# Retention and a mixture of experts: 18 chunks of 128 tokens in place of 24 chunks of 96

## The chip, the core and the metric

The kernel runs on one NeuronCore of a Trainium2 chip. The metric is the device time of one execution in microseconds (us), the median over runs. The core has five engines that run side by side and meet only through semaphores: TensorE (PE, matrix products; PEld is its loading of stationary operands), VectorE (DVE), ScalarE (ACT), GpSimd (POOL) and SyncE (SP, which here only issues DMAs). SBUF is the on-chip memory, PSUM the eight banks into which TensorE writes.

## The reference

```
scores = q @ k.T / sqrt(64)                       # 4 batches, 8 heads, 576 tokens, 64 dims
gamma  = 1 - 2 ** (-5 - head)
ret    = scores * (rel >= 0 ? gamma ** rel : 0)   # rel = query position - key position
x      = (ret @ v), heads side by side            # 2304 tokens x 512
logits = x @ w_gate                               # 8 experts
expert = argmax(logits);  gate = 1 / sum(exp(logits - max))
slot of a token = how many tokens before it chose the same expert (capacity 576)
out[token] = gate * relu(x[token] @ w1[expert]) @ w2[expert]     # 512 -> 1024 -> 512
```

The sequences are independent in the retention; the count of the slots runs over all 2304 tokens in order.

## The kernel before

**Retention.** A batch of 576 tokens is cut into NC = 6 chunks of C = 96 tokens. Instead of the whole score matrix the kernel keeps a running state of each head, the sum of k times v over all earlier chunks of the sequence, with k divided by its decay. For chunk c of batch b TensorE does, in this order:

- `inter` (L483, 8 matmuls): state times the decayed q, `qs`; left out where c is 0. It waits for `qs_made` and `state_copied`.
- `intra` (L493, 8): v times the masked scores `probs`. It waits for `masked`.
- `add_state` (L501, 8): scaled k (`k_sc`) times v, added up in PSUM bank 6; left out in the last chunk of a batch.
- `scores` of the next chunk (L469, 8).
- `turn_chunk` (L512, 4 transposes) and `gate_logits` (L519, 4 matmuls of 8 columns against `w_gate`).

Every one of these is a product in full float32, which the profile shows as two matmul records each (transposes: one), so `inter` is x16. The eight matmuls of a group work in pairs on two halves of the array. Moving columns are the tokens of a chunk, except in `add_state` (64) and in the transposes (128); the stationary operand of `scores`, `turn_chunk` and `gate_logits` has as many columns as the chunk has tokens, that of the others 64.

Beside it, GpSimd makes `qs` (L366: q times a decay table `q_dec`, one table for each of the chunk positions, loaded in five DMAs during the first batch) and `k_sc` (L371). VectorE makes `probs` (L860, `mask`: scores in PSUM times a table in `const`, two instructions a chunk) and copies the logits (L864). ScalarE copies x out of PSUM (L732, `xT`), copies the state out of PSUM in two instructions of 64 partitions (L751) and copies the turned x (L738, `x_nat`), which SyncE stores to `x_rows` in DRAM. When a chunk has been turned, SyncE issues the loads of q and k (`qk_raw`) and of k and v (`kv_raw`) of the chunk three ahead, into one of three buffers.

**Routing.** Six chunks make a routing group, here a batch. While the next batch runs, VectorE picks the experts (`pick_expert`), TensorE counts (`count_before`, L528, L531, L534), VectorE makes slots and payloads (`positions`, `pay_rows`, `slots`, `pay_gates`) and TensorE adds the group to a map of slots (`make_map`, L545). The last group is routed in two parts, four chunks early and two after the end of the retention, and ends in index tables.

**Experts.** Then GpSimd gathers the rows of each expert, and each expert runs 16 blocks of 12 matmuls (L634 to L636), its weights split by ScalarE (L727) and VectorE (L851) into a high and a low part. This stage follows from the routing alone.

**Loops.** `by_batch` writes out the first and the last batch and runs batches 1 and 2 in one loop with registers. The order on each engine is the order of the code.

Of the kernel before, what the change touches and what calls it, by code (L numbers as in the profile page):

```python
# [35 lines left out]
ZERO_STEPS = 12  # L36
# [18 lines left out]
K_RANK = K_DK + NC * HEADS  # L55
# [7 lines left out]
def shape_constants():  # L63

    gamma = 1.0 - 2.0 ** (-5.0 - np.arange(HEADS))
    pos = np.arange(SEQ).reshape(NC, C).T
# [7 lines left out]
    k[:, K_IOTA:K_ALL] = np.arange(CAP)  # L74
    k[:, K_DK:K_RANK] = (gamma ** -pos[:, :, None].astype(np.float64)).reshape(C, -1)
# [7 lines left out]
    qd = gamma[head][:, None, :, None] ** np.arange(SEQ) / np.sqrt(DH)  # L83
    qd = np.broadcast_to(qd, (2, DH, PAIRS, SEQ)).reshape(128, PAIRS, NC, C).transpose(0, 2, 1, 3)
# [9 lines left out]
def by_batch(eng, body):  # L94

    body(0, True, False)
    with eng.Fori(1, BATCH - 1) as b:
        body(b, False, False)
    return body(BATCH - 1, False, True)
# [20 lines left out]
def retention_moe(nc, qk, kv, w_gate, w1, w2, consts, qdecay, eye, out):  # L120
# [6 lines left out]
    with ExitStack() as ctx:  # L127
# [25 lines left out]
        with ExitStack() as one:  # L153
# [7 lines left out]
            q_dec = s1("q_dec", [128, NC, PAIRS, C])  # L161
# [60 lines left out]
        q_dec_in = [sem(f"q_dec_in{c}") for c in range(NC)]  # L222
# [64 lines left out]
        def _(sp):  # L287
            def load_chunk(b, c):
                sp.dma_start(qk_raw[:, c % 3], qk[b, c]).then_inc(qk_in[c % 3], 16)
                sp.dma_start(kv_raw[:, c % 3], kv[b, c]).then_inc(kv_in[c % 3], 16)  # L290
# [13 lines left out]
            def load_decay(c):  # L304
                sp.dma_start(q_dec[:, c], qdecay[:, c]).then_inc(q_dec_in[c], 16)

            sp.dma_start(qk_raw[:, 0], qk[0, 0]).then_inc(qk_in[0], 16)
            sp.dma_start(const[:, 0:K_RANK], consts[:, 0:K_RANK]).then_inc(const_in, 16)
            sp.dma_start(kv_raw[:, 0], kv[0, 0]).then_inc(kv_in[0], 16)
            sp.dma_start(qk_raw[:, 1], qk[0, 1]).then_inc(qk_in[1], 16)  # L310
# [7 lines left out]
            def batch(b, first, last):  # L318
                for c in range(NC):

                    sp.wait_ge(x_turned, b * NC + c + 1)
                    if not (last and c + 3 >= NC):
                        load_chunk(b + (c + 3) // NC, (c + 3) % NC)
                    sp.wait_ge(x_copied, b * NC + c + 1)
                    sp.dma_start(x_rows[bass.ds((b * NC + c) * C, C), :], x_nat[:, c % 2, :]
                                 ).then_inc(x_stored[c % 2], 16)
                    if first and c + 3 < NC:
                        load_decay(c + 3)
# [6 lines left out]
            by_batch(sp, batch)  # L335
# [14 lines left out]
        def _(pool):  # L350
# [7 lines left out]
            def scale_chunk(b, c):  # L358
                n = b * NC + c

                wait(pool, x_made, n - 1)
                wait(pool, state_made, b * (NC - 1) + max(c - 1, 0))
                if c > 0:
                    pool.wait_ge(q_dec_in[c], 16)
                    pool.wait_ge(qk_in[c % 3], 16 * (2 * b + c // 3 + 1))
                    pool.tensor_tensor(qs[:, c % 2], qk_raw[:, c % 3, 0], q_dec[:, c], ALU.mult  # L366
                                       ).then_inc(qs_made, 1)
                if c < NC - 1:
                    pool.wait_ge(kv_in[c % 3], 16 * (2 * b + c // 3 + 1))
                    decay = const[:, K_DK + c * HEADS:K_DK + (c + 1) * HEADS].unsqueeze(2).broadcast_to((C, HEADS, DH))  # L370
                    pool.tensor_tensor(k_sc[:, c % 2], kv_raw[:, c % 3, 0], decay, ALU.mult).then_inc(k_scaled, 1)  # L371
# [757 lines left out]
```

## Time and profile before

| | us |
|---|---|
| median of 3 runs | 385.71 |
| lowest, highest | 381.7, 389.11 |
| the profiled execution | 387.06 |
| its span, first to last instruction | 385.1 |
| TensorE busy | 358.6 |
| VectorE busy | 214.5 |
| ScalarE busy | 186.8 |
| GpSimd busy | 135.0 |

A row of the timeline or of the chain of waits begins with start and length in us from the span's start. In the chain, the pieces lie end to end: each is what the end of the kernel waited for at that moment. A row of a stretch gives its length, the busy time of each engine with the number of its instructions, the granted TensorE clock, the DMA engines' busy share and GB/s.

### The profile page before, as it was taken

What the parts mean: (1) busy time and instruction counts of PE and PEld (TensorE: products, weight loads), DVE (VectorE), ACT (ScalarE), POOL (GpSimd) and SP (SyncE); (2) the same over time, 40 slices, a digit from 0 to 9 for tenths busy, and PEclk for the clock granted to TensorE, in tenths of its full rate; (3) what the DMA queues carried; (4) which work ended last, traced back from release to release, by engine and by line L of the source; (5) the groups of instructions that cost most, each with busy time, mean ns of one, the idle gap of its engine ahead of it and who ended that gap; (6) DMA issues with size and microseconds to landing.
All of it is one profiled execution on the core that took longest, in us unless ns stands there. A gap on an engine that the chain in (4) does not pass through costs nothing.

```text
span 385.1 us, 10982 instructions
## 1 busy us (share of the span) xinstructions
PE 358.6 (93%) x3594; PEld 338.4 (88%) x3595; DVE 214.5 (56%) x450; ACT 186.8 (48%) x367; POOL 135.0 (35%) x131
## 2 busy tenths in 40 slices
PE   8999999999999799499899999989999999998993
PEld 4998888999976599399899999989999999998992
DVE  3145545838774475356456556646756757754741
ACT  1344343436431365266365447547657646655641
POOL 3675344534506223025205504522542541321323
PEclk9999999999995999799999999999999999999999
DMA  8789987887963599815635544654663664550101
GB/s 240 222 267 270 307 248 216 248 255 218 272 192 109 185 386 372 311 61 190 196 111 176 167 163 129 202 184 136 204 220 136 202 211 136 197 163 4 60 0 56
DMA packets 27435, 73.41 MB, mean 191 GB/s; under 512 B 7114, under 2 KB 7882, under 8 KB 27408
## 3 DMA queue, kind: packets, MB, share of 16 engines
q1 hardware_dynamic: 21008, 63.57, 51.2%
q0 software_dynamic: 6400, 9.46, 8.2%
q8 instruction: 18, 0.29, 0.3%
q14 instruction: 9, 0.07, 0.1%
HBM read 64.61 MB, written 19.92 MB: 220 GB/s over the span
## 4 chain that ended last, share of the span: by engine, by line
PE 85%; issue 5%; DVE 3%; DMA 3%; POOL 2%; ACT 1%; POOLq 0%; another core or an unknown queue 0%; DVEq 0%; ACTq 0%; SPq 0%
PE bank L634 18%; PE bank L636 18%; PE bank L635 17%; PE bank L469 5%; PE bank L483 4%; PE bank L493 4%; PE bank L519 4%; PE bank L512 3%; PE bank L627 3%; PE bank L622 3%; PE bank L501 2%; DMA qk_raw<-in_qk 2%; PE bank L572 1%; DMA x_gat<-x_rows,slot_row 1%; PE bank L545 1%
## 5 line engine op out<-in xcount | busy, mean ns | idle before, releaser
L634 PE MATMUL bank<-m_hi,w_hi 128*128 x512 | 155.1, 303 | 6.5 <-DVE w_lo L851 3.2
L635 PE MATMUL bank<-m_hi,w_lo 128*128 x512 | 153.7, 300 | 0.0
L636 PE MATMUL bank<-m_lo,w_hi 128*128 x512 | 153.1, 299 | 0.0
L851 DVE TENSOR_TENSOR w_lo<-w_raw,w_hi 128x512 fp32r<-128x512 f32 x128 | 89.0, 695 | 37.2 <-ACT w_hi L727 33.6
L634 PEld LDWEIGHTS bank<-m_hi,w_hi 128*128 128x128 f32 x512 | 96.2, 188 | 10.1 <-issue 10.1
L635 PEld LDWEIGHTS bank<-m_hi,w_lo 128*128 128x128 f32 x512 | 96.2, 188 | 0.0
L636 PEld LDWEIGHTS bank<-m_lo,w_hi 128*128 128x128 f32 x512 | 96.2, 188 | 0.0
L727 ACT ACTIVATE w_hi<-w_raw 128x512 fp32r<-128x512 f32 x128 | 79.6, 625 | 25.0 <-PE bank L636 21.1
L388 POOL DMA_INDIRECT out<-y_nat,slot_row x40 | 41.7, 1042 | 133.6 <-PE bank L636 87.1
L1030 DVE SCALAR_TENSOR_TENSOR m_lo<-bank,m_hi 128x384 fp32r<-128x384 f32 x64 | 35.7, 558 | 38.8 <-ACT m_hi L809 35.8
L382 POOL DMA_INDIRECT x_gat<-x_rows,slot_row x37 | 40.4, 1093 | 46.2 <-PE bank L636 27.5
L809 ACT ACTIVATE m_hi<-bank 128x384 fp32r<-128x384 f32 x64 | 31.5, 492 | 40.8 <-PE bank L636 37.5
L860 DVE TENSOR_TENSOR probs<-bank,const 96x384 f32<-96x384 f32 x48 | 24.4, 548 | 40.5 <-PE bank L469 40.4
L366 POOL TENSOR_TENSOR qs<-qk_raw,q_dec 128x384 f32<-128x384 f32 x20 | 20.8, 1039 | 34.8 <-DMA qk_raw<-in_qk 21.8
L732 ACT ACTIVATE xT<-bank 128x384 f32<-128x384 f32 x24 | 11.8, 490 | 39.1 <-PE bank L493 39.1
L788 ACT ACTIVATE y_sb<-bank 128x384 f32<-128x384 f32 x32 | 15.7, 491 | 30.4 <-PE bank L636 27.2
L371 POOL TENSOR_TENSOR k_sc<-kv_raw,const 96x512 f32<-96x512 f32 x20 | 20.8, 1041 | 19.9 <-DMA kv_raw<-in_kv 19.9
L738 ACT ACTIVATE x_nat<-bank 96x512 f32<-96x512 f32 x24 | 14.2, 592 | 25.6 <-PE bank L512 23.0
L1042 DVE TENSOR_TENSOR y_sb<-bank,y_sb 128x384 f32<-128x384 f32 x32 | 17.8, 557 | 13.3 <-PE bank L636 11.1
L766 ACT ACTIVATE m_hi<-bank 128x512 f32 (+1 forms) x24 | 13.3, 598 | 24.2 <-PE bank L622 13.9
L1026 DVE TENSOR_TENSOR m_lo<-bank,m_hi 128x512 f32 (+1 forms) x24 | 15.5, 687 | 16.7 <-ACT m_hi L766 15.5
L469 PE MATMUL bank<-qk_raw 64*96 64x96 f32 x384 | 23.7, 266 | 0.7 <-DMA qk_raw<-in_qk 0.7
(89 smaller groups left out, 360.7 us busy)
## 6 DMA issues: line engine op xcount, KB each, us to landing
w_raw<-in_moe_w SPq DMA_DIRECT2D x64, 512.0 KB, 3.3
qk_raw<-in_qk SPq DMA_DIRECT2D x24, 384.0 KB, 4.7
kv_raw<-in_kv SPq DMA_DIRECT2D x24, 384.0 KB, 5.3
x_rows<-x_nat SPq DMA_DIRECT2D x24, 192.0 KB, 4.5
out<-zeros SPq DMA_DIRECT2D x12, 384.0 KB
q_dec<-in_qdecay SPq DMA_DIRECT2D x5, 192.0 KB, 5.2
out<-y_nat,slot_row POOLq DMA_INDIRECT x40, 2.7
x_gat<-x_rows,slot_row POOLq DMA_INDIRECT x37, 2.9
```

The lines of the kernel that those rows point to most:

```text
L366: pool.tensor_tensor(qs[:, c % 2], qk_raw[:, c % 3, 0], q_dec[:, c], ALU.mult).then_inc(qs_made, 1)
L382: pool.indirect_dma_start(out=dst[:, g, :], out_offset=None, in_=x_rows[:, :], in_offset=bass.IndirectOffsetOnAxis(ap=slot_row[:, g, e:e + ...
L388: pool.indirect_dma_start(out=out[:, :], out_offset=bass.IndirectOffsetOnAxis(ap=slot_row[:, g, e:e + 1], axis=0), in_=y_nat[:, g, :], in_ ...
L469: last = pe.matmul(score_ps[0:C, u, p * C:(p + 1) * C], qk_raw[r, c % 3, 1, p, :], qk_raw[r, c % 3, 0, p, :], start=True, stop=True, skip_ ...
L634: pe.matmul(dst, w_hi[:, s, i, :], hi[:, i, cols], start=(i == 0), stop=False)
L635: pe.matmul(dst, w_lo[:, s, i, :], hi[:, i, cols], start=False, stop=False)
L636: last = pe.matmul(dst, w_hi[:, s, i, :], lo[:, i, cols], start=False, stop=(i == K4 - 1))
L727: act.activation(w_hi[:, j % SLOTS], w_raw[j // 2][:, j % 2 * 512:j % 2 * 512 + 512].rearrange("p (k n) -> p k n", k=K4), ACT.Copy).then_i ...
L809: last = act.activation(m_hi[:, H0 + j, 0:WA], ring[j % SLOTS][:, 0:WA], ACT.Relu)
L851: dve.tensor_tensor(w_lo[:, j % SLOTS], w_raw[j // 2][:, j % 2 * 512:j % 2 * 512 + 512].rearrange("p (k n) -> p k n", k=K4), w_hi[:, j % S ...
L860: dve.tensor_tensor(probs[:, u], src, decay[:, u], ALU.mult).then_inc(masked, 1)
L1030: return dve.scalar_tensor_tensor(out=m_lo[:, H0 + f, cols], in0=src, scalar=0.0, in1=m_hi[:, H0 + f, cols].bitcast(f32), op0=ALU.max, op1 ...
```

## The change

The chunk grows from 96 to 128 tokens, so that 2304 tokens are 18 chunks. 576 is 4.5 x 128, so the chunks run over sequence ends: nine chunks (`PERIOD`) hold two sequences, and in the fifth of them (`MID`, chunks 4 and 13) the first 64 tokens end one sequence and the last 64 begin the next. There the mask is made in three pieces per half (a memset of zeros, 64 rows x 4x64, and 64 rows x 512), `inter` takes 64 columns only, and the state starts anew. `inter` is left out in chunks 0 and 9, `add_state` in chunks 8 and 17.

Six chunks are still a routing group, so there are three groups instead of four. The group loop is written out in full on every engine.

`q_dec` becomes one table of 128x512 for all chunks, loaded once; what a chunk's start adds to the decay is put into the state: VectorE multiplies the state by a column of `const` while it copies it from PSUM (`scale_state`, two instructions of 64x4x64), and ScalarE's state copies go. The first load of `const`, for which the mask and `k_sc` wait, becomes 128x1132 elements.

```diff
-C = 96
-NC = SEQ // C
+C = 128
+CHUNKS_ALL = TOKENS // C
+NC = 6
+GROUPS = CHUNKS_ALL // NC
+PERIOD = 2 * SEQ // C
+MID, HALF = SEQ // C, SEQ % C
...
-ZERO_STEPS = 12
+ZERO_STEPS = 9
...
-            q_dec = s1("q_dec", [128, NC, PAIRS, C])
+            q_dec = s1("q_dec", [128, PAIRS, C])
...
-            load_decay(1)
-            sp.dma_start(kv_raw[:, 1], kv[0, 1]).then_inc(kv_in[1], 16)
-            load_chunk(0, 2)
-            load_decay(2)
...
+            sp.dma_start(q_dec[:, :, :], qdecay).then_inc(q_dec_in, 16)
+            sp.dma_start(kv_raw[:, 1], kv[1]).then_inc(kv_in[1], 16)
+            load_chunk(2)
...
-                    if first and c + 3 < NC:
-                        load_decay(c + 3)
...
-            def scale_chunk(b, c):
-                n = b * NC + c
-
+            def scale_chunk(n):
+                c = n % PERIOD
                 wait(pool, x_made, n - 1)
-                wait(pool, state_made, b * (NC - 1) + max(c - 1, 0))
+                wait(pool, state_made, with_state(n - 2))
                 if c > 0:
-                    pool.wait_ge(q_dec_in[c], 16)
-                    pool.wait_ge(qk_in[c % 3], 16 * (2 * b + c // 3 + 1))
-                    pool.tensor_tensor(qs[:, c % 2], qk_raw[:, c % 3, 0], q_dec[:, c], ALU.mult
+                    cols = slice(0, HALF if c == MID else C)
+                    if n == 1:
+                        pool.wait_ge(q_dec_in, 16)
+                    pool.wait_ge(qk_in[n % 3], 16 * (n // 3 + 1))
+                    pool.tensor_tensor(qs[:, n % 2, :, cols], qk_raw[:, n % 3, 0, :, cols], q_dec[:, :, cols], ALU.mult
                                        ).then_inc(qs_made, 1)
...
-                    if c < NC - 1:
-
-                        act.wait_ge(state_made, b * (NC - 1) + c + 1)
-                        if first and c == 0:
-                            act.wait_ge(zero_made, 2)
-                        for u in range(2):
-                            r = slice(64 * u, 64 * u + 64)
-                            last_copy = act.activation(state[r, :, r], state_ps[r, :, :], ACT.Copy)
-                        last_copy.then_inc(state_copied, 1)
-                    copy_x(b, c)
+                    copy_x(n)
...
+                parts = ((slice(0, C), slice(0, C)),)
+                if n % PERIOD == MID:
+                    parts = ((slice(0, HALF), slice(0, HALF)), (slice(HALF, C), slice(0, C)))
                 for u in range(2):
-                    src = score_ps[0:C, u, 0:PAIRS * C].rearrange("c (a i) -> c a i", a=PAIRS)
-                    dve.tensor_tensor(probs[:, u], src, decay[:, u], ALU.mult).then_inc(masked, 1)
+                    if n % PERIOD == MID:
+                        dve.memset(probs[0:HALF, u, :, HALF:C], 0.0)
+                    for rows, cols in parts:
+                        src = score_ps[rows, u, :].rearrange("c (a i) -> c a i", a=PAIRS)[:, :, cols]
+                        last = dve.tensor_tensor(probs[rows, u, :, cols], src, decay[rows, u, :, cols], ALU.mult)
+                    last.then_inc(masked, 1)
+
+            def scale_state(n):
+
+                start = K_SS + (n + 1) % PERIOD * PAIRS
+                dve.wait_ge(state_made, with_state(n))
+                for u in range(2):
+                    r = slice(64 * u, 64 * u + 64)
+                    last = dve.tensor_tensor(state[r, :, r], state_ps[r, :, :],
+                                             const[r, start:start + PAIRS].unsqueeze(2).broadcast_to((64, PAIRS, DH)),
+                                             ALU.mult)
+                last.then_inc(state_copied, 1)
...
+                    if n % PERIOD < PERIOD - 1:
+                        scale_state(n)
+                return link
```

TensorE's queue in the first batch, before the change: `inter`, `intra`, `add_state`, then the next chunk's `scores`, the transposes and the logits (the shape is output partitions x moving columns).

```order
L483 MATMUL bank<-qs,state 64x96 x8
L493 MATMUL bank<-probs,kv_raw 64x96 x8
L501 MATMUL bank<-kv_raw,k_sc 64x64 x8
L469 MATMUL bank<-qk_raw 96x96 x8
L512 MATMUL bank<-ident,xT 96x128 x4
L519 MATMUL bank<-wg,xT 96x8 x4
```

The same queue in the changed kernel, from the end of chunk 3 through chunk 4, the one over a sequence end.

```order
L529 MATMUL bank<-wg,xT 128x8 x4
L492 MATMUL bank<-qs,state 64x64 x8
L502 MATMUL bank<-probs,kv_raw 64x128 x8
L511 MATMUL bank<-kv_raw,k_sc 64x64 x8
L476 MATMUL bank<-qk_raw 128x128 x8
L522 MATMUL bank<-ident,xT 128x128 x4
L529 MATMUL bank<-wg,xT 128x8 x4
L492 MATMUL bank<-qs,state 64x128 x8
```

The order of a chunk's work stands as it was; what is wider is the moving side of three groups and the stationary side of three.

VectorE's queue before, in the second and third chunk of the first batch: masks and the copy of the logits of the chunk before.

```order
L860 TENSOR_TENSOR probs<-bank,const 96x384 x2
L864 COPY logits<-bank 96x8
L860 TENSOR_TENSOR probs<-bank,const 96x384 x2
L864 COPY logits<-bank 96x8
L860 TENSOR_TENSOR probs<-bank,const 96x384 x2
```

VectorE's queue in the changed kernel, from chunk 2 to the end of chunk 4's mask.

```order
L868 TENSOR_TENSOR probs<-bank,const 128x512 x2
L884 COPY logits<-bank 128x8
L877 TENSOR_TENSOR state<-bank,const 64x4x64 x2
L868 TENSOR_TENSOR probs<-bank,const 128x512 x2
L884 COPY logits<-bank 128x8
L877 TENSOR_TENSOR state<-bank,const 64x4x64 x2
L865 MEMSET probs 64x4x64
L868 TENSOR_TENSOR probs<-bank,const 64x4x64
L868 TENSOR_TENSOR probs<-bank,const 64x512
L865 MEMSET probs 64x4x64
L868 TENSOR_TENSOR probs<-bank,const 64x4x64
L868 TENSOR_TENSOR probs<-bank,const 64x512
```

Two state instructions have come in between the logits' copy of one chunk and the mask of the next; where a chunk has routing work (from the second group on), that work stands ahead of them.

## Rows read from the trace of the kernel before

**Rows 1.** The page's first part: busy time, share of the span, instructions.

```profile
PE 358.6 (93%) x3594; PEld 338.4 (88%) x3595; DVE 214.5 (56%) x450; ACT 186.8 (48%) x367; POOL 135.0 (35%) x131
```

**Rows 2.** Stretches: length, PE, PEld, DVE, ACT, POOL busy; clock, DMA share, GB/s.

```profile
0.00:18.50 18.50, 16.75 (x134) 12.32 (x137) 4.10 (x9) 4.13 (x9) 9.24 (x14) 1.00 0.78 224
18.50:110.50 92.00, 88.83 (x1640) 83.08 (x1636) 55.27 (x165) 39.91 (x89) 40.48 (x37) 1.00 0.86 254
110.50:131.00 20.50, 17.24 (x120) 11.49 (x120) 9.75 (x39) 4.42 (x8) 7.68 (x8) 0.75 0.46 137
131.00:385.00 254.00, 235.74 (x1704) 231.55 (x1704) 145.34 (x238) 138.31 (x262) 77.63 (x73) 0.98 0.50 170
```

**Rows 3.** Chain of waits, one chunk of the last batch: start, length, piece.

```profile
91.19 0.81 PE bank L483 x16
92.00 0.66 PE bank L493 x16
92.66 0.47 PE bank L501 x16
93.12 0.85 PE bank L469 x16
93.97 0.57 PE bank L512 x4
94.55 0.60 PE bank L519 x8
```

**Rows 4.** Chain of waits: a cold chunk's piece, a stall, map, batch start, count.

```profile
16.03 1.28 PE bank L493 x16
...
32.27 0.47 issue
...
84.25 0.97 PE bank L545 x9
...
87.27 0.88 PE bank L493 x16
...
89.47 0.15 PE bank L528
...
90.10 0.48 PE bank L512 x4
```

**Rows 5.** Waits, 0 to 131 us: engine, line, waited for, total, times, longest.

```profile
PE bank L469 <- DMA qk_raw<-in_qk: 0.7, 1, 0.7
...
PE bank L528 <- DVE onehot L896: 0.9, 2, 0.6
```

**Rows 6.** Groups by line and shape: out<-in, count, busy us, mean ns, idle before.

```profile
L860 DVE TENSOR_TENSOR probs<-bank,const 96x384 f32<-96x384 f32 x48 | 24.4, 548 | 40.5 <-PE bank L469 40.4
...
L1026 DVE TENSOR_TENSOR m_lo<-bank,m_hi 128x512 f32 x21 | 13.4, 686 | 14.6 <-ACT m_hi L766 14.5
...
L751 ACT ACTIVATE state<-bank 64x256 f32<-64x256 f32 x40 | 15.1, 378 | 1.7 <-PE bank L501 1.5
...
L371 POOL TENSOR_TENSOR k_sc<-kv_raw,const 96x512 f32<-96x512 f32 x20 | 20.8, 1041 | 19.9 <-DMA kv_raw<-in_kv 19.9
L366 POOL TENSOR_TENSOR qs<-qk_raw,q_dec 128x384 f32<-128x384 f32 x20 | 20.8, 1039 | 34.8 <-DMA qk_raw<-in_qk 21.8 <-DMA q_dec<-in_qdecay 8.9 <-PE bank L501 4.1
```

**Rows 7.** Timeline, VectorE and GpSimd side by side: start, length, instruction.

```profile
37.36 1.04 POOL L371 TENSOR_TENSOR k_sc<-kv_raw,const 96x512 f32<-96x512 f32 x1 [0.43 <-DMA kv_raw<-in_kv]
37.50 0.96 DVE L896 TENSOR_TENSOR onehot<-ranked,r_max 96x48 bf16<-96x48 f32 x1
```

**Rows 8.** Two stretches with full DMA queues, and the page's row on a load.

```profile
36.30:49.00 12.70, 11.76 (x225) 11.07 (x224) 8.27 (x30) 5.00 (x13) 5.11 (x6) 1.00 1.02 311
...
141.00:151.00 10.00, 9.76 (x78) 9.55 (x77) 7.25 (x12) 5.76 (x12) 5.34 (x5) 1.00 1.00 357
...
qk_raw<-in_qk SPq DMA_DIRECT2D x24, 384.0 KB, 4.7
```

**Rows 9.** Timeline at the start: first k_sc and first intra.

```profile
7.17 1.03 POOL L371 TENSOR_TENSOR k_sc<-kv_raw,const 96x512 f32<-96x512 f32 x1 [4.62 <-DMA kv_raw<-in_kv]
...
8.46 1.55 PE L493 MATMUL bank<-probs,kv_raw 96*64 96x96 f32 x16
```

More of the change, by code:

```diff
@@ L91, in wait, with by_group, with_state @@
         eng.wait_ge(sem, value)
[L94 to L99, printed above, removed]
+def by_group(body):
+    for g in range(GROUPS):
+        link = body(g, g == 0, g == GROUPS - 1)
+    return link
+def with_state(n):
+    return n + 1 - (n + 1) // PERIOD
 def by_count(eng, count, body, large, sizes=None):
@@ L221, in retention_moe @@
         out_zeroed = sem("out_zeroed")
-        q_dec_in = [sem(f"q_dec_in{c}") for c in range(NC)]
+        q_dec_in = sem("q_dec_in")
         gate_in = sem("gate_in")
@@ L334, in batch @@
                         load_weights(0, c)
-            by_batch(sp, batch)
+            by_group(group)
             sp.wait_ge(xs_tr, 2 * NA)
@@ L580, in _, with group @@
             pe.wait_ge(scores_cleared, 1)
-            scores(0, 0)
+            scores(0)
             keep_warm(1)
-            def batch(b, first, last):
+            def group(b, first, last):
                 for c in range(NC):
                     n = b * NC + c
-                    inter(b, c)
-                    intra(b, c)
-                    if c < NC - 1:
-                        add_state(b, c)
-                    elif not first and not last:
+                    inter(n)
+                    intra(n)
+                    if n % PERIOD < PERIOD - 1:
+                        add_state(n)
+                    if c == NC - 1 and not first and not last:
                         make_map(b - 1)
-                    if not (last and c == NC - 1):
-                        scores(b + (c + 1) // NC, (c + 1) % NC)
+                    if n + 1 < CHUNKS_ALL:
+                        scores(n + 1)
                     if not first and c == 0:
@@ L732, in copy_xT, with copy_x, group @@
                 act.activation(xT[:, :, :], xT_ps, ACT.Copy).then_inc(xT_copied, 1)
-            def copy_x(b, c):
-                act.wait_ge(x_turned, b * NC + c + 1)
-                wait(act, x_stored[c % 2], 16 * (b * NC // 2 + c // 2))
-                act.activation(x_nat[:, c % 2, :], x_ps[0:C, :], ACT.Copy).then_inc(x_copied, 1)
-            def batch(b, first, last):
+            def copy_x(n):
+                act.wait_ge(x_turned, n + 1)
+                wait(act, x_stored[n % 2], 16 * (n // 2))
+                act.activation(x_nat[:, n % 2, :], x_ps[0:C, :], ACT.Copy).then_inc(x_copied, 1)
+            def group(b, first, last):
                 for c in range(NC):
@@ L759, in batch @@
                         w_high(0, 2 * c + 1)
-            by_batch(act, batch)
-            act.wait_ge(dif_made, BATCH + 1)
+            by_group(group)
+            act.wait_ge(dif_made, GROUPS + 1)
             act.activation(l_exp[:, :, :], l_dif[:, :, :], ACT.Exp).then_inc(exp_made, 1)
@@ L965, in cast_tables, with group @@
                 dve.wait_ge(const_cast, 4)
-            def batch(b, first, last):
+            def group(b, first, last):
+                link = None
                 for c in range(NC):
```

144 lines of the change are left out of this document (75 added, 69 removed).

## The prediction

> **What bounds the kernel now.** I read the busy shares first: TensorE is busy for 358.6 of 385.1 us, VectorE for 214.5 [rows 1]. Then the stretches. The retention runs to about 110.5 us, the last routing to 131, the experts to the end; in the 92 us from 18.5 to 110.5 TensorE is busy for 88.8 us and the DMA engines for 86% at 254 GB/s [rows 2]. So in the stage that the change touches TensorE sets the pace and the DMA engines come second. The experts (254 us) keep their code and data, and I take them as unchanged. Last the chain of waits. One warm chunk is six pieces of TensorE without a gap: 0.81 + 0.66 + 0.47 + 0.85 + 0.57 + 0.60 = 3.96 us [rows 3]. Up to about 18.5 us the same pieces take almost twice that, `intra` 1.28 us for 0.66 [rows 4, 3]: TensorE is at its lower clock there, whatever the clock column says for a stretch without a record. The stalls in the chain are small: 0.47 us without a visible waiter at 32.27, where `inter` stands ready and its last input, `qs`, had itself waited for a table `q_dec` [rows 4, 6]; 0.9 us for the one-hot of VectorE; 0.7 us once for a `qk_raw` load [rows 5].
>
> **The change, part by part.**
>
> *Wider chunks on TensorE.* `intra` and `add_state` have equal tiles and differ in moving columns, 96 against 64: 0.66 against 0.47 us [rows 3]. So 32 columns on eight matmuls cost 0.19 by the difference and 0.22 in proportion; I take 0.21. From it, at 128:
> `inter` 0.81 + 0.21 = 1.02; `intra` 0.66 + 0.21 = 0.87; `add_state` stays 0.47 (it moves 64 columns still; only the contraction is longer); the transposes stay 0.57, plus 0.01 for a wider first load. `scores` moves and loads 128 for 96: 0.85 + 0.21 = 1.06 if only moving columns count, 1.13 if all of it scales by 4/3; I take 1.11. `gate_logits` moves 8 columns only, so its 0.60 is weight loads of 96 columns: 0.60 if a load's time does not grow, 0.80 at 4/3; no row shows wide loads of this kind alone, and I take 0.80, since with 8 moving columns nothing else is left to fill the time.
> A chunk is then 1.02 + 0.87 + 0.47 + 1.11 + 0.58 + 0.80 = 4.85 us, 22% longer for 33% more tokens. The gain is what does not grow: `add_state`, the transposes, and the first latency of each group.
> Before: 24 x 3.96 = 95.0, less four `inter` and four `add_state` (0.81 + 0.47), plus 0.22 at each batch's start, where `intra` takes 0.88 for 0.66 [rows 4]: 90.8. After: 18 x 4.85 = 87.3; chunks 0 and 9 save 1.02 - 0.22 each, chunks 8 and 17 save 0.47 each, chunks 4 and 13 have an `inter` of 64 columns, 0.60, and save 0.42 each: 87.3 - 1.6 - 0.9 - 0.8 = 84.0. **Gain 6.8 us.** With loads that cost nothing it would be 6.8 + 18 x 0.25 = 11.3; with all four scaled groups and the transposes at 4/3 a chunk is 4.94 + 0.18, and the gain 2.0.
>
> *One routing group less.* A map costs 0.97 us, a count 90.10 - 89.47 = 0.63 less the 0.09 that the next transpose is shorter [rows 4]. **Gain 1.5.**
>
> *Stalls that go.* One `q_dec` in place of five tables that come with the chunks: the 0.47 at 32.27 goes. The one-hot was late because VectorE works on it for some 2.1 us after a chunk's logits while TensorE needs only `intra`, `add_state`, `scores` to reach the count; after, an `inter` comes first (the group starts at chunks 6 and 12 are not sequence starts) and the pieces are longer, 3.5 us in all: the 0.9 goes [rows 5]. The load stall of 0.7 may stay. **Gain 1.4.**
>
> *The state on VectorE.* ScalarE's two copies of 378 ns leave a queue that is not on the path. VectorE gets two of 256 elements: its time from PSUM is 548 ns at 384 and 686 at 512 [rows 6], so some 420 at 256, 0.8 a pair; the masks go from 548 to 686 each, about 1.3 a pair. From the end of `add_state` to the next `inter` TensorE has 1.11 + 0.58 + 0.80 = 2.5 us of other work, VectorE needs 0.9: hidden by 1.6 us. The next mask may start when `scores` are done, 1.1 us after `add_state`, just when the state is finished; `intra` comes 0.58 + 0.80 + 1.02 = 2.4 us later and the mask needs 1.3. Behind routing work: the one-hot chain (2.1) plus state (0.8) ends 2.9 us after the logits, where `inter` comes at 4.85. In the last group a chunk has up to 2.1 of gates and a weight split of 0.7 (rows of VectorE's kind at 686 ns [rows 6]) ahead of its state: 3.7, still ahead of 4.85. What takes this cover away is GpSimd: the one-hot of 0.2 us took 0.96 where it met `k_sc` (37.36 to 38.40), ending when that ended [rows 7]. A split that meets `qs` (1.04 x 4/3 = 1.4 us) gives up to 1.4 once or twice in the last group. I put 0 to 3 us in all, and take 0.6.
>
> *The middle chunks.* Two memsets and four products replace two: 2 x (0.2 + 0.4 + 0.6) = 2.4 us, and chunk 4's `intra` comes 0.58 + 0.80 + 0.60 = 2.0 us after its scores. A stall of 0.4 to 0.5, at chunk 4; chunk 13 has a count (0.6) between and hides it. **Loss 0.5.**
>
> *Loads.* A chunk brings 0.52 + 0.52 + 0.26 = 1.31 MB per 4.85 us, 270 GB/s, for 0.98 MB per 3.96 us before, 248. The queues have carried 311 and 357 GB/s when full [rows 8]. A load has the time of two chunks less the pieces after `scores`, about 8.0 us for 6.6 before, and took 4.7 [rows 8]; 4/3 of it is 6.3. No change, with 0 to 8 us as the bounds (below).
>
> *Start and tail.* The first `k_sc` waits for `kv_raw` at 7.17, the first `intra` runs at 8.46 behind warming matmuls [rows 9]. Before it must land 1.60 MB for 1.08; at the 360 GB/s of a full queue that is 1.5 us later, 8.6, so 0.2 is lost. In the part at the lower clock both kernels work without a break, about six warm microseconds each. The tail's `xT` copy and logits grow by 0.3. **Loss 0.5.**
>
> Sum: 6.8 + 1.5 + 1.4 - 0.6 - 0.5 - 0.5 = 8.1 us. The profiled execution took 387.06, so it would take 379.0; it lies 1.35 above the median of 385.71, so the median becomes 377.6, which I round to 377.5.
>
> A rule that speaks against the move of the state is in the Trainium skill, "TensorEngine Tiling (Array Packing)", Performance Considerations, PSUM Bottleneck: use both ScalarE and VectorE to empty PSUM. By that rule VectorE is the next bound, which is the third rival below.
>
> **The rivals.**
> - *The DMA engines bind.* Against my figure of 270 GB/s stands their 86% at 254 GB/s [rows 2], which extrapolates to 295 at full. If they could in truth give no more than now, the stage's 23.4 MB take 92 us as before, and all that is left is nothing to 2 us of routing: 384 to 386. At 295 they take 79 us and do not bind on average, but loads come late in bursts (the two weight loads of the first group): 2 to 4 us, 380 to 382. For it: 0.7 us of it are there already [rows 5]. Against: 311 and 357 [rows 8]. Chance 0.25, most of it the mild form.
> - *Loads of weights don't grow* with the columns, or the wider groups start sooner: up to 4.5 us more gain, 373. Chance 0.12.
> - *VectorE binds (slower).* Each chunk's `inter` or `intra` waits for VectorE because state, split and masks are held by GpSimd. It cancels the gain from 8.1 / 18 = 0.45 us of stall per chunk; slower by 2% needs 0.9 us in every chunk, 393.4. The cover of 1.6 us and of 1.1 us speaks against it. Chance 0.07.
> - *The clock.* The part at the lower clock ends at about 18.5 us now; every microsecond that it lasts longer costs half of that. If TensorE falls back to it in the retention for 10 us, 5 us are lost: 382.5. Nothing between 18.5 and 110.5 shows it [rows 2]. Chance 0.06.
>
> **How the numbers follow.** My forecast has the remaining 0.50. Its own range is 375 to 380.5. With the rivals, 372.5 to 384 leaves out about 2 in 10. Faster by over 2%, about what a measurement of this kernel can tell from no change, is below 378.0: the better half of the forecast and the second rival, 0.54 with the runs' scatter. Within 2%: 0.39. Slower: 0.07.
>
> **What would show it.** In the profile after: chunk pieces of about 1.02, 0.87, 0.47, 1.11, 0.58, 0.80 in the chain, the retention done near 102 us; no wait for `q_dec` or for the one-hot; a mask wait at chunk 4 only; DMA share near 0.9. Wrong if a chunk takes 5.3 us or more (all scales by 4/3), if waits for `qk_raw` or for `state_copied` come in many chunks, or if the experts' 254 us move by more than 2.

## The result, and the profile after

The change takes the median from 385.71 to 372.46 us: ratio 0.969, 95% interval 0.962 to 0.977. The forecast was 377.5, in the range 372.5 to 384. So the direction was right and the gain, 13.2 us, is well over the 8.1 that the sum gave. The ratio is of the fast runs alone (one of the old kernel's five was slow), and by it the gain is 11.8 us and the new time 373.9. That is inside the range, while the plain median, 372.46, lies on its lower edge. The profiled execution took 374.73 (span 372.9) beside 387.06 (span 385.1) before, and the difference of these two spans, 12.2 us, is what the rows below can account for.

The page of the kernel after, busy time (as [rows 1]) and its row on the load of q and k (as the last of [rows 8]):

```profile
PE 348.2 (93%) x3178; PEld 330.3 (89%) x3179; DVE 219.1 (59%) x447; ACT 168.2 (45%) x314; POOL 129.1 (35%) x123
...
qk_raw<-in_qk SPq DMA_DIRECT2D x18, 512.0 KB, 4.7
```

Stretches of the kernel after (columns as in [rows 2]: PE, PEld, DVE, ACT, POOL, clock, DMA share, GB/s):

```profile
0.00:18.50 18.50, 16.48 (x176) 12.80 (x179) 7.79 (x16) 3.90 (x7) 11.05 (x16) 1.00 0.88 317
18.50:96.00 77.50, 74.66 (x1180) 70.11 (x1178) 54.94 (x154) 20.25 (x36) 33.38 (x28) 1.00 0.83 273
96.00:118.00 22.00, 18.93 (x127) 13.18 (x123) 10.06 (x41) 4.91 (x9) 7.20 (x7) 0.69 0.45 136
118.00:372.90 254.90, 238.09 (x1704) 234.15 (x1704) 146.27 (x238) 139.13 (x262) 77.43 (x73) 0.97 0.50 169
```

The retention ends near 96 us and not near 102; the two stages behind it are slightly longer than before (22.0 for 20.5, 254.9 for 254.0). A warm chunk in the chain of waits of the kernel after, to be read against [rows 3]:

```profile
53.90 1.09 PE bank L476 x16
54.99 0.59 PE bank L522 x4
55.58 0.79 PE bank L529 x8
56.38 1.02 PE bank L492 x16
57.40 0.87 PE bank L502 x16
58.27 0.47 PE bank L511 x16
```

These are `scores`, transposes, `gate_logits`, `inter`, `intra`, `add_state`: 4.83 us for the forecast 4.85, each piece within 0.02. TensorE's waits in the retention (8.3 to 96 us), line, what it waited for, total, times, longest:

```profile
PE bank L502 <- DVE probs L868: 2.6, 4, 1.2
...
PE bank L492 <- DVE state L877: 0.4, 1, 0.4
```

There is no wait for `q_dec`, for the one-hot or for a load any more; in their place `intra` waits for VectorE's masks four times (0.28 of the 2.6 us is the very first one) and `inter` once for the state.

**Where the 12.2 us lie.** I cut both spans at three places that both kernels pass: the start of the `intra` of the chunk that begins at token 384 (chunk 4 before, chunk 3 after; 384 is a multiple of both sizes), the last matmul of the last `intra`, and the experts' first product with `w_hi`. The forecast column sorts the prediction's own terms into the same parts.

The two rows on which the first part rests, before and after:

```profile
28.94 0.83 PE L493 MATMUL bank<-probs,kv_raw 96*64 96x96 f32 x16
...
23.25 1.04 PE L502 MATMUL bank<-probs,kv_raw 128*64 128x128 f32 x16
```

| part | before | after | gained | forecast |
|---|---|---|---|---|
| to the `intra` at token 384 | 28.94 | 23.25 | 5.7 | 1.1 |
| from it to the last `intra` | 80.78 | 72.76 | 8.0 | 8.0 |
| to the experts' first matmul | 21.42 | 21.96 | -0.5 | -1.1 |
| experts | 253.9 | 254.9 | -1.0 | 0 |
| span | 385.1 | 372.9 | 12.2 | 8.0 |

(Forecast: 4 chunks of 3.96 against 3 of 4.85 are 1.3, less 0.2 at the start; 19 chunk steps against 14 are 6.2, a group 1.5, stalls +1.4 and -1.1; the last chunk's wider pieces 0.8 and the tail 0.3.) The steady part is right as a sum. The gain that was not forecast is in the first quarter of the retention. The expert row flatters the change: a second trace of the old kernel has 251.1 us there, without the 3.2 us of waits for `w_lo` that the first one has, and against it the new kernel's experts are 3.8 us longer.

### The profile page after: what moved, and what is told of

The parts are those of the page before. It is cut to its first block, busy times and chain, and to the rows that moved or that the text cites. A ratio compares the mean times of both kernels' runs of the same rounds, so it can differ in the third digit from the quotient of the medians.

```text
span 372.9 us, 9780 instructions
## 1 busy us (share of the span) xinstructions
PE 348.2 (93%) x3178; PEld 330.3 (89%) x3179; DVE 219.1 (59%) x447; ACT 168.2 (45%) x314; POOL 129.1 (35%) x123
## 4 chain that ended last, share of the span: by engine, by line
PE 89%; DVE 4%; issue 4%; DMA 1%; ACT 1%; POOL 1%; POOLq 0%; DVEq 0%; ACTq 0%
PE bank L644 20%; PE bank L645 19%; PE bank L646 19%; PE bank L476 5%; PE bank L502 4%; PE bank L632 4%; PE bank L492 4%; PE bank L529 3%; PE bank L637 3%; PE bank L522 2%; DVE probs L868 2%; PE bank L511 2%; PE bank L582 2%; DMA y_nat<-x_rows,slot_row 1%; DVE y_sb L1065 1%
## 5 line engine op out<-in xcount | busy, mean ns | idle before, releaser
L395 POOL DMA_INDIRECT out<-y_nat,slot_row x40 | 40.1, 1002 | 137.9 <-PE bank L646 106.1
L389 POOL DMA_INDIRECT x_gat<-x_rows,slot_row x37 | 41.3, 1118 | 43.6 <-PE bank L646 18.1
L868 DVE TENSOR_TENSOR probs<-bank,const 128x512 f32<-128x512 f32 (+2 forms) x40 | 25.1, 660 | 8.8 <-PE bank L476 8.6
L742 ACT ACTIVATE xT<-bank 128x512 f32<-128x512 f32 x18 | 10.7, 597 | 42.9 <-PE bank L502 42.9
L373 POOL TENSOR_TENSOR qs<-qk_raw,q_dec 128x512 f32<-128x512 f32 (+1 forms) x16 | 19.8, 1236 | 27.9 <-DMA qk_raw<-in_qk 20.4
L877 DVE TENSOR_TENSOR state<-bank,const 64x256 f32<-64x256 f32 x32 | 13.5, 422 | 18.3 <-PE bank L511 18.0
L748 ACT ACTIVATE x_nat<-bank 128x512 f32<-128x512 f32 x18 | 10.7, 597 | 29.3 <-PE bank L522 29.3
L476 PE MATMUL bank<-qk_raw 64*128 64x128 f32 x288 | 21.8, 293 | 0.0
```

The costliest lines, as they stand in the source:

```text
L389: pool.indirect_dma_start(out=dst[:, g, :], out_offset=None, in_=x_rows[:, :], in_offset=bass.IndirectOffsetOnAxis(ap=slot_row[:, g, e:e + ...
L395: pool.indirect_dma_start(out=out[:, :], out_offset=bass.IndirectOffsetOnAxis(ap=slot_row[:, g, e:e + 1], axis=0), in_=y_nat[:, g, :], in_ ...
L476: last = pe.matmul(score_ps[0:C, u, p * C:(p + 1) * C], qk_raw[r, n % 3, 1, p, :], qk_raw[r, n % 3, 0, p, :], start=True, stop=True, skip_ ...
L868: last = dve.tensor_tensor(probs[rows, u, :, cols], src, decay[rows, u, :, cols], ALU.mult)
```

## The experiments

### At the start: the clock, the loads or the tables

Before, TensorE was at its lower level (1.2 GHz) until 18.5 us: its matmuls take twice as long [rows 4]. After, the record of the granted clock steps to the full level at 7.6 us, and the first `intra` is at full speed from the start. Timeline of the kernel after, its first `intra` (before it took 1.55 [rows 9]):

```profile
8.70 1.09 PE L502 MATMUL bank<-probs,kv_raw 128*64 128x128 f32 x16 [0.28 <-DVE probs L868]
```

The new kernel's warming matmuls run on 128 rows and not 96, so that was the first suspect. One run gives the old kernel wide warming, one the new kernel narrow warming.

```diff
-        zeros = sb("zeros", [C, TOKENS // ZERO_STEPS // C * D])
+        zeros = sb("zeros", [128, TOKENS // ZERO_STEPS // C * D])
...
-                    pe.matmul(unused[0:C, 0:n], zeros[:, 0:C], zeros[:, 0:n], start=True, stop=True,
+                    pe.matmul(unused[0:128, 0:n], zeros[:, 0:128], zeros[:, 0:n], start=True, stop=True,
```

> The kernel before, with nothing changed but its warming products of zeros: they use 128 rows and 128 columns of the array in place of 96 and 96 (the tile of zeros is 128 partitions high). Theory A1 (the wider warming products raise the clock earlier): the clock is up near 8 us instead of 18.5, first intra at 8.5, and 4 to 5 us are saved, ratio 0.987. Theory A2 (the wider chunk's own products do it) or B (luck): the rise stays at about 18.5 us or moves in either direction over executions, ratio 1.00.

Measured: 387.1 us, ratio 1.002 (0.998 to 1.007). The clock rose at 5.4 us (at 6.4 in a second trace), and the kernel gained nothing.

```diff
-                    pe.matmul(unused[0:C, 0:n], zeros[:, 0:C], zeros[:, 0:n], start=True, stop=True,
+                    pe.matmul(unused[0:96, 0:n], zeros[0:96, 0:96], zeros[0:96, 0:n], start=True, stop=True,
```

> The changed kernel with its warming products cut back to 96 rows and 96 columns. Theory A1: the clock rises later than 12 us and 3 to 5 us are lost against after_again. Theory A2: the rise stays near 8 us and nothing is lost, within 1 us of after_again.

Measured: 376.74 us, ratio 0.973 (0.964 to 0.981), beside 375.89 for the unchanged new kernel on the same chip. The clock rose at 8.9 us: narrow warming does not hold it down. So wide warming goes with an early rise in the old kernel, but the new one doesn't need it, and by itself it is worth nothing in time.

> The changed kernel unchanged, for its scatter. Theory A (the clock's early rise comes with the change): the clock is up before 12 us again, the warm chunk is 4.82 us again, chunks 4 and 13 stall on VectorE again, ratio to the kernel before 0.962 to 0.977. Theory B (the early rise was luck of that execution): the clock rises anywhere from 7 to 19 us, and the time is up to 5 us longer when it is late.

Measured: 375.89 us, ratio 0.975 (0.969 to 0.980); the clock rose at 6.5 us, the `intra` at token 384 came at 23.00.

A further run makes only one half of the change: chunks stay at 96, but there is one decay table, and VectorE puts the chunk's start into the state.

```diff
-                sp.dma_start(q_dec[:, c], qdecay[:, c]).then_inc(q_dec_in[c], 16)
+            sp.dma_start(q_all[:, :], qdecay).then_inc(q_dec_in, 16)
...
-                                last_copy = act.activation(state[r, :, r], state_ps[r, :, :], ACT.Copy)
+                    last = dve.tensor_tensor(state[r, :, r], state_ps[r, :, :],
+                                             starts[r, at:at + PAIRS].unsqueeze(2).broadcast_to((64, PAIRS, DH)),
+                                             ALU.mult)
```

> The kernel before with only the second half of the change: one decay table for q, and VectorE multiplies the state by the decay of a chunk's start while it copies it. Chunks stay 96 tokens, loops and groups stay. Theory: TensorE's pieces stay 3.96 us a chunk, the 0.47 us at 32 us goes, VectorE's state copy is hidden outside the routing chunks and costs 0 to 2 us in the last batch: ratio 0.997 to 1.005, clock rise at about 18.5. Rival (VectorE binds): 0.4 us or more in most of the 20 chunks with a state, ratio over 1.02.

Measured: 389.41 us, ratio 1.007 (1.002 to 1.011). The clock rose at 8.6 us with narrow warming and narrow chunks.

What each of these gave at the start can be read from 9 to 20 us (columns as in [rows 2]). The kernel before:

```profile
9.00:20.00 11.00, 11.00 (x132) 10.44 (x128) 1.94 (x5) 3.28 (x8) 6.20 (x5) 1.00 0.78 224
```

Before with wide warming, and from its timeline an `inter` and the `qs` that it waited for:

```profile
9.00:20.00 11.00, 9.46 (x170) 8.65 (x170) 2.36 (x6) 3.90 (x9) 5.54 (x5) 0.96 1.04 257
...
16.51 0.99 POOL L366 TENSOR_TENSOR qs<-qk_raw,q_dec 128x384 f32<-128x384 f32 x1 [2.96 <-DMA q_dec<-in_qdecay]
17.60 0.88 PE L483 MATMUL bank<-qs,state 128*64 128x96 f32 x16 [1.28 <-issue]
```

96-token chunks with one table:

```profile
9.00:20.00 11.00, 10.38 (x197) 9.63 (x194) 5.06 (x13) 2.65 (x5) 7.65 (x7) 1.00 1.04 257
```

The kernel after:

```profile
9.00:20.00 11.00, 11.00 (x185) 10.51 (x183) 4.62 (x11) 2.88 (x5) 9.50 (x8) 1.00 0.96 336
```

In the first row TensorE is busy all the time but at the lower clock (132 matmul records in 11 us), and in this trace the DMA engines have slack, 0.78 (a second trace of the old kernel has 0.97 there, and TensorE idles in neither). Once the clock is up the old kernel's demand outruns them: 257 GB/s at a share of 1.04, and TensorE idles 1.5 us of 11, 1.28 of it at once, behind `qs` behind a table. A second trace of that kernel has 4.2 us in three such waits before token 384. So the lower clock hid slow loads, and the earlier clock alone gave nothing in the total. Without four of the five tables (0.8 MB) the idle time falls to 0.6 us. The wide kernel moves 336 GB/s in the same stretch and never waits. The `intra` at token 384 comes at 28.94 in the old kernel (29.96 in another trace of it), 27.76 (with a fall of the clock on the way, 19.0 to 22.4 us) and 29.53 with wide warming, 25.49 with one table, 23.25 with the whole change.

So of the 5.7 us some 3.5 go with the earlier clock and the fewer table bytes together (the clock alone gave nothing in the total; fewer bytes at the lower clock had no run), and some 2.2 with the wide chunks, 1.3 of that TensorE's own. These shares are rough: each stands on one or two traces, and the two of the old kernel differ by 1.0 us.

### The experts

TensorE waits twice for "issue" inside the experts, at the first transposes of an expert, where the old kernel waits once. Waits from 118 us on, kernel after:

```profile
PE bank L632 <- issue: 8.3, 2, 5.6
```

The same in the kernel before (from 131 us; its L622 is the same operation):

```profile
PE bank L622 <- issue: 5.6, 1, 5.6
```

The diff doesn't touch that stage, but it writes the group loop out in full on every engine. One run does that alone to the kernel before:

```diff
-    body(0, True, False)
-    with eng.Fori(1, BATCH - 1) as b:
-        body(b, False, False)
-    return body(BATCH - 1, False, True)
+    for b in range(BATCH):
+        link = body(b, b == 0, b == BATCH - 1)
+    return link
```

> The kernel before with only its loop over batches 1 and 2 written out, as the change does it. Theory: registers and branches cost TensorE the stalls without a waiter near 51 and 60 us, 0.9 us, so 0.5 to 1.5 us faster than before, ratio 0.997. Rival (nothing of the gain comes from the loops): ratio 1.000 within its interval; or more instructions to fetch cost up to 1 us.

Measured: 389.25 us, ratio 1.017 (1.008 to 1.026), 5.9 us over the old kernel's 383.39 on the same chip, where 0.5 to 1.5 us less was expected. Its waits from 117 us on, on the corresponding line:

```profile
PE bank L621 <- issue: 8.1, 2, 5.6
```

The second stall is there, in a kernel that differs only in the written-out loop; the kernels with the loop written out have it (7.3 to 8.4 us in two waits; one further below, which routes its tokens otherwise, has the second wait on another line), the five traces of looped 96-token kernels have one, of 5.5 to 5.9. What the extra stall is, the timeline of the kernel after shows, and its DMA queues from 180 to 186 us:

```profile
185.17 2.18 PE L632 MATMUL bank<-ident,x_gat 128*128 128x128 f32 x9 [2.70 <-issue]
...
q8 instruction: 2, 0.03, 2.0%
```

The expert's transposes start 2.7 us late, and two packets of instructions arrive in that stretch, the second of them from 184.2 us on, just ahead of the stall's end. A second trace of the old kernel has one such packet at its corresponding place, 193 to 199 us:

```profile
q8 instruction: 1, 0.02, 1.2%
```

The Trainium skill, "Runtime: NRT & Kernel Launch", Instruction fetch mechanics, says that instructions come in blocks of 16 KiB and that a taken branch to a target outside the window stalls until the block has come, and prefers full unrolling for that. The trace agrees with the block size (0.03 MB in two packets) and with a stall where the expert loop starts again; the advice did not hold here, since unrolling one loop brought a stall in another. That TensorE waited for that packet, and that the code's place against the blocks decides it, is argued; the runs show only that the stall comes with the written-out loop. Behind it the granted clock falls to half for 3.4 us in the kernel after (185.1 to 188.5 us, mean 0.50), another 1.7 us at most. In the old kernel with the loop written out the retention was 1.5 us longer too, with 2.3 us of waits for `qk_raw` for 0.7 [rows 5]; why, no run shows. Beside the second trace of the old kernel (span 382.1 for 387.6) its retention is 1.3 us longer and its experts 4.3, which is nearly the whole 5.9; the stall is 2.5 of the 4.3, and further short waits for "issue" are 1.6.

### VectorE: the state and the middle chunks

The stall at chunk 4 in the chain of waits of the kernel after, from `scores` to `intra`:

```profile
24.76 1.12 PE bank L476 x16
25.97 0.27 DVE probs L865
26.26 0.42 DVE probs L868
26.69 0.69 DVE probs L868
27.49 0.27 DVE probs L865
27.77 0.42 DVE probs L868
28.20 0.71 DVE probs L868
28.91 0.14 issue
29.05 1.09 PE bank L502 x16
```

The mask in three pieces per half runs 2.94 us from end to end. TensorE's other work is `turn_chunk`, `gate_logits` and a 64-column `inter`, and `intra` is 1.2 us late. Chunk 13 repeats it, and chunk 14 follows. Timeline, kernel after:

```profile
73.66 1.09 PE L502 MATMUL bank<-probs,kv_raw 128*64 128x128 f32 x16 [0.91 <-DVE probs L868]
...
75.36 1.27 POOL L373 TENSOR_TENSOR qs<-qk_raw,q_dec 128x512 f32<-128x512 f32 x1 [2.72 <-PE bank L511]
75.47 1.70 DVE L852 TENSOR_TENSOR w_lo<-w_raw,w_hi 128x512 fp32r<-128x512 f32 x1
77.10 0.85 DVE L877 TENSOR_TENSOR state<-bank,const 64x256 f32<-64x256 f32 x2
78.09 1.09 PE L492 MATMUL bank<-qs,state 128*64 128x128 f32 x16 [0.40 <-DVE state L877]
...
79.41 1.09 PE L502 MATMUL bank<-probs,kv_raw 128*64 128x128 f32 x16 [0.22 <-DVE probs L868]
```

The late mask pushes logits, positions and the weight split `w_lo` behind it; `w_lo` meets GpSimd's `qs` and takes 1.70 us for 0.70; the state after it is late by 0.4 and the next mask by 0.2. In one run the middle chunks are masked like any other (the zeros between the two sequences are left out):

```diff
-                if n % PERIOD == MID:
-                    parts = ((slice(0, HALF), slice(0, HALF)), (slice(HALF, C), slice(0, C)))
...
-                    if n % PERIOD == MID:
-                        dve.memset(probs[0:HALF, u, :, HALF:C], 0.0)
```

> The changed kernel with chunks 4 and 13 masked like all others, two products a chunk (the zeros between two sequences are left out of the mask). Theory: the two stalls of 1.2 and 0.9 us that the traces show before intra of chunks 4 and 13 go, and chunk 14's with them: 2 to 3 us faster than after_again, ratio 0.968. Rival (the stalls are made up for behind, as TensorE is fed by others later): under 1 us.

Measured: 370.18 us, ratio 0.967 (0.961 to 0.973). From the first `intra` to the last matmul of the last it takes 84.65 us, for 87.31 and 87.05 in the two traces of the unchanged kernel without a clock fall in that stage; and one mask wait of 0.4 us is left. So the middle chunks cost 2.4 to 2.7 us, their followers counted, where the forecast had 0.5.

The other half of the question is the state. Here ScalarE copies it, as before, without the decay of the chunk's start:

```diff
+                        for u in range(2):
+                            r = slice(64 * u, 64 * u + 64)
+                            last_copy = act.activation(state[r, :, r], state_ps[r, :, :], ACT.Copy)
...
-                    if n % PERIOD < PERIOD - 1:
-                        scale_state(n)
```

> The changed kernel with the state copied by ScalarE in two instructions as before, and not multiplied by the decay of a chunk's start (this part of the computation is left out). It frees VectorE of 32 instructions of 422 ns, 13.5 us busy. Theory (VectorE's late mask and state at chunks 13 and 14 cost 1.8 us, and half of the change by itself costs the 2.6 us that c96_scale_state lost): 2 to 3 us faster than after_again, about 373.5 in the same company, ratio 0.967. Rival (the state's move is hidden, c96_scale_state lost its 2.6 us otherwise): within 1 us of after_again, ratio 0.975.

Measured: 384.6 us, ratio 1.005. The total says nothing: with x scaled wrongly the routing sends the tokens elsewhere, and the experts take 267 us for 255. The retention alone can be read, 86.1 us for 87.05 to 87.31: the state on VectorE costs about 1 us, near the forecast 0.6. In the 96-token kernel with the state on VectorE the cover is thinner. Three of its waits of TensorE, 8.3 to 112 us:

```profile
PE bank L484 <- DVE state L861: 0.9, 3, 0.5
...
PE bank L494 <- DVE probs L852: 0.5, 3, 0.2
PE bank L529 <- DVE onehot L900: 0.5, 1, 0.5
```

The first two, 1.4 us, the old kernel does not have. From token 384 to the last `intra` it takes 82.5 us for 80.8, so 1.7 of the 3.5 us that the start gave are taken back, and the retention still ends 1.7 us earlier than before. Even so the whole is 0.7% slower. In its trace that lies in the experts, whose code is the same: 259.1 us for 254.0, with 5.0 us of waits for `w_lo` where the old kernel has 3.2 in one trace and none in the other. So this half of the change does not pay by itself, but the state's move is not shown to be the reason; why those waits grow, no run shows.

### Both repaired

If the masks and the state cost what the two runs say, both can be had back without changing the result. ScalarE copies the state with the decay as its scale operand (eight instructions of 64x64, since the scale is one column a head pair), and the middle chunks use a second table with the zeros in it, so that their mask is two instructions like any other:

```diff
+                        for u in range(2):
+                            r = slice(64 * u, 64 * u + 64)
+                            for p in range(PAIRS):
+                                last_copy = act.activation(state[r, p, r], state_ps[r, p, :], ACT.Copy,
+                                                           scale=const[r, at + p:at + p + 1])
...
+                at = K_MID if n % PERIOD == MID else K_MASK
...
-                    if n % PERIOD < PERIOD - 1:
-                        scale_state(n)
```

> The changed kernel with both of VectorE's burdens taken off it and the computation kept: ScalarE multiplies the state while it copies it, in eight instructions of 64x64 with a scale per partition, and chunks 4 and 13 are masked in two products against a second table, which comes with the second load of const (0.5 MB more). Theory: ScalarE needs some 1.6 to 2.0 us for the eight, which the 2.5 us from add_state to the next inter cover; no mask stall is left: 2.5 to 4 us faster than after_again, ratio 0.965. Rival: the eight copies take more than 2.4 us and every inter waits for them: 0.5 us x 16 or more lost, ratio 0.99.

Measured: 369.27 us, ratio 0.964 (0.958 to 0.971). ScalarE's group in the retention (8 to 94 us), and the waits of TensorE that are left:

```profile
L767 ACT ACTIVATE state<-bank,const 64x64 f32<-64x64 f32 x128 | 29.1, 303 | 0.5
...
PE bank L506 <- DVE probs L883: 0.5, 1, 0.5
PE bank L480 <- DMA qk_raw<-in_qk: 0.4, 1, 0.4
```

Eight copies are 2.4 us of ScalarE for each chunk and TensorE never waits for them. Then the new kernel and this one side by side on one chip, with two single runs of the old one, the second with wide warming:

> The kernel of best, beside after_pair. Theory (the middle chunks' mask and VectorE's state are worth 2.7 us of retention, as the traces of after_again 87.05 and best 84.30 show): 2.5 to 4.5 us under after_pair, and retention from first to last intra 84.3 us. Rival (a good half of the 0.9644 was its chip): under 2 us.

> The changed kernel again, on the same chip as best_pair and two looks at the kernel before. Expected by all theories: 0.970 to 0.977 of the kernel before, retention from first to last intra 87 us, the clock up before 10 us.

> The kernel before, unchanged, for when its clock rises. Theory A (the lower clock up to 18.5 us belongs to this kernel, and the change shortens it): the rise is again at 18 to 19 us. Theory B (luck of the execution): it is elsewhere, as near 8 us.

> The kernel before with warming products of 128 rows and columns, a second look at its clock. Theory A1: up near 5 to 8 us again, and retention 2 to 5 us shorter than in the kernel before. Theory B: anywhere between 5 and 19 us. It also shows whether the fall at 19.0 us that its first trace has comes again.

Measured: 368.32 (0.957, 0.949 to 0.965) against 374.77 (0.972, 0.963 to 0.981), so the repaired kernel is 6.4 us faster than the new one, more than the 2.5 to 4.5 of the theory. Retention 84.1 for 89.1 us; the experts, which the edit does not touch, take 252.5 for 254.9, so not all of the 6.4 is the repair's. The old kernel took 384.08 with its clock up at 20.7 us; with wide warming it took 386.92, its clock up at 6.4 us.

The 89.1 of the new kernel here holds something that its other two traces have not. Around the stall at chunk 4 its clock falls. One stretch of that trace:

```profile
28.50:32.00 3.50, 3.50 (x45) 3.38 (x41) 2.22 (x6) 0.60 (x1) 1.96 (x3) 0.52 0.62 224
```

The same stretch with the middle chunks masked like the others:

```profile
28.50:32.00 3.50, 3.50 (x57) 3.29 (x54) 3.06 (x7) 1.19 (x2) 1.65 (x2) 1.00 0.83 300
```

Granted 0.52 for 1.00: half speed for 3.4 us, 1.7 us lost. With narrow warming the new kernel had it too, at 29.4; so two of five traces with that stall (the kernel after in three traces, its narrow-warmed twin and the one with ScalarE's copies), none of the three of the new layout in which the mask is whole. The old kernel with wide warming has it at 19.0 and 30.3 us, after its own stalls behind `qs`. That the stalls bring it fits every case, but the same stall went by without it in three traces.

## Why the prediction was right, and where its sizes were wrong

- **Wider chunks on TensorE: right.** The six pieces came within 0.02 us each, and from token 384 on TensorE's busy time fell by 78.15 - 69.92 = 8.2 us, for 7.7 from the chunks and the group. Weight loads do grow with the columns: `gate_logits` took 0.79 for the 0.80 at 4/3, which ends that rival.
- **Stalls that go: right, and under-sized.** 2.6 us were there (the 0.7 for a load, the second "issue" of 0.5 that I had not listed, and the two that I had), and all went, for 1.4.
- **The state on VectorE: right.** 422 ns for 420; about 1 us in all for 0.6. The collision of a split with `qs` that I named came, once.
- **The middle chunks: the step that was most wrong in the steady part.** "A stall of 0.4 to 0.5, at chunk 4": it was 1.2, and 0.9 at chunk 13. The sum of the mask was 2.4 and it took 2.94: the memset is 0.27 for 0.2, the 64x512 product 0.70 for 0.6 (half the partitions save nothing against 686 ns at 128), and there are gaps between the pieces, 0.16 in all, 0.11 of it between the two halves. "Chunk 13 has a count between and hides it": the count's three pieces there take 0.3 us of TensorE and not 0.6, and I had not asked what stands behind the late mask on VectorE. 2.4 to 2.7 us for 0.5.
- These two errors, +1.2 and -1.6 in the stalls, nearly cancel, and TensorE's work fell by 0.5 more than forecast, so that the steady part's 8.0 us came out as forecast: partly luck.
- **The start: the term that was mis-sized, and the largest miss.** "In the part at the lower clock both kernels work without a break, about six warm microseconds each." I took the clock's rise as a fixed time of the chip, and it is not: it came at 4.6 to 8.9 us in every kernel but the old looped and unrolled ones with narrow warming and five tables, at 18.5 to 20.7 there. A part forecast at 1.1 gave 5.7, by the rise and the loads and the wide chunks together.
- **The DMA rival: fell.** No wait for a load came in the retention of the profiled run (one of 0.6 us in a second trace), at 317 GB/s up to 18.5 us and 273 after it, with the share down from 0.86 to 0.83, where I had 0.9. The rival took the 86% at 254 GB/s for a measure of room that wider chunks keep; the same share carries more bytes now.
- **The clock rival: not in the profiled run, but real.** "Nothing between 18.5 and 110.5 shows it" held for one trace. It came in two of five traces and costs 1.7 us.
- **Experts that should not "move by more than 2": kept, 1.0, by luck.** There was a cause to find, a stall of 2.7 us brought by the written-out loop, and the old kernel's profiled run happened to be long there: against its second trace they moved by 3.8. The price of unrolling stood nowhere in my sum.
- **The total: right in direction, and only just in size.** 372.5 was the range's lower bound, and the forecast's own part of it ended at 375. What carried the time below that, the start, was none of the rivals; the rival with the same time in it, loads of weights that don't grow, did not happen.

Open: why the clock rose late in just those three traces. The old kernel with wide warming, the one with one table and the new one with narrow warming all had an early rise, so none of wide warming, one table and wide chunks is needed for it. Chance of the execution is not excluded: the one-table kernel and the old one run the same matmuls at the same times up to the first `intra` at 8.46 us, and the clock rises at 8.6 us in one and at 18.5 in the other. And how the 2.7 us of stall could have been avoided was not tried: the new kernel with a loop would need its two kinds of chunk in one body.

## What to carry over

Where a stage is made of pieces with a fixed cost, price a size change piece by piece from a warm chunk's chain; TensorE's pieces came out to a few per cent. Then do the same for the small instructions of the engine that is second: count each with the row of its own shape, put what waits behind them in the queue into the sum, and prefer a bigger table to a special case in three pieces. And treat two things as part of the change even where the diff doesn't name them: the first microseconds, where a clock that comes up earlier shows whatever loads it had been hiding, and the written-out code, which brought a stall into a stage that nobody touched.

## What the runs showed of the hardware that I had not expected

**DMA rate and chunk shape.** From 9 to 20 us, with full queues, 96-token chunks moved 239 to 257 GB/s (three traces of two kernels, with and without the tables) and 128-token chunks 336 to 355 (three traces). Kernel before, the long stretch, against the second row of the kernel after above:

```profile
18.50:96.00 77.50, 74.87 (x1382) 70.28 (x1380) 43.20 (x128) 33.64 (x76) 35.61 (x33) 1.00 0.87 256
```

A share of 0.87 for 256 GB/s before, 0.83 for 273 after: 12% more bytes for each busy share. Two things change with the chunk, the partitions that a transfer of `kv_raw` or x reaches (96 or 128) and the length of a packet of `qk_raw` (384 KB, or 512, over 128 partitions: 3072 or 4096 bytes), and no run tells them apart. Packets of the same 4096 bytes took 274 ns each in the old kernel with wide warming and 192 in the new one, 9 to 20 us, so length is not all of it. The Trainium skill, "SBUF — State Buffer", Door 1: The DMA port swizzle, says that the rate depends on how many of 16 ports the partitions reach, with partitions 0 to 63 on the even ports and 64 to 127 on the odd ones. By that rule 96 partitions load the even ports twice as much as the odd ones and take as long as 128, which would give 0.75 of the rate if all transfers were such. But `qk_raw` and `q_dec` have 128 partitions in both kernels, and only some half of the bytes in that stretch go to or from 96; so the rule's ratio is about 0.86 here (an estimate), and 257 to 336 is 0.76. The rule may be a part of the difference, and no run shows how large a part; the old kernel reached 311 GB/s where weight loads ran among the others [rows 8].

**Eight small copies on ScalarE cost TensorE nothing here.** 303 ns for 64x64 with a scale column, against 378 for 64x256 without: a quarter of the elements saves a fifth of the time, so eight copies are 2.4 us of the engine for the 0.8 of two, and TensorE still never waited for them.

**Half the partitions, the same time.** Groups of VectorE in the retention of the kernel after, by shape:

```profile
L868 DVE TENSOR_TENSOR probs<-bank,const 128x512 f32<-128x512 f32 x31 | 20.0, 686 | 4.5 <-PE bank L476 4.4
...
L877 DVE TENSOR_TENSOR state<-bank,const 64x256 f32<-64x256 f32 x32 | 13.5, 422 | 18.3 <-PE bank L511 18.0
...
L868 DVE TENSOR_TENSOR probs<-bank,const 64x512 f32<-64x512 f32 x4 | 2.8, 695 | 0.1
```

The columns set the time: 695 ns on 64 partitions, 686 on 128.
